# A mixture's transposes and logits put beside attention's last eight chunks, its weights given places of their own, and its other half written anew

## The reference

```python
# 1: linear attention with the delta rule; q, k, v: (4, 8, 768, 48)
for t in range(S):
    y[:, :, t] = einsum('bhd,bhde->bhe', q[:, :, t], state)
    v_old = einsum('bhde,bhd->bhe', state, k_n[:, :, t])
    state = state + beta_t * einsum('bhd,bhe->bhde', k_n[:, :, t], v_t - v_old)
x = y.transpose(0, 2, 1, 3).reshape(3072, 384)
# 2: soft mixture of 8 experts with 4 slots each
logits = x @ phi                                   # (3072, 32)
d = softmax(logits, axis=0)                        # over the tokens
slot_input = d.T @ x                               # (32, 384)
slot_out[e] = relu(slot_input[e] @ w1[e]) @ w2[e]  # w1 (8, 384, 1024), w2 (8, 1024, 384)
x = softmax(logits, axis=1) @ slot_out
# 3: feed-forward
h = x @ w_in                                       # w_in (384, 2048)
out = (h * sigmoid(1.702 * h)) @ w_out             # w_out (2048, 384)
```

## Time and profile before

| stage | from, us | to, us |
|---|---|---|
| attention, chunks 0 to 15 | 0 | 186.5 |
| attention, chunks 16 to 19 | 186.5 | 219.7 |
| attention, chunks 20 to 23 | 219.7 | 252.8 |
| transposes of x and logits | 252.8 | 291.6 |
| maxima, exponential, slots' inputs | 291.6 | 306.4 |
| experts, stacks, product with w_in | 306.4 | 360.3 |
| feed-forward | 360.3 | 590.2 |

### The profile page before, as it was taken

One profiled execution on the slowest core, in us unless ns is written; L12 is line 12 of the kernel. 1 busy time (PEld: TensorE's weight loads), 2 busy tenths in 40 slices (PEclk: granted clock), 3 DMA queues, 4 the chain that ended last, 5 costly groups with the idle time before them and its releaser, 6 DMA issues. The chain is left out here.

```text
span 590.2 us, 17597 instructions
## 1 busy us (share of the span) xinstructions
PE 488.2 (83%) x7320; PEld 354.7 (60%) x7320; DVE 364.7 (62%) x1139; ACT 281.6 (48%) x595; POOL 39.4 (7%) x50
## 2 busy tenths in 40 slices
PE   5537879788887777669898675999999999999997
PEld 4415556556554455447533323887878878788786
DVE  3997889979898981012312646655656556565563
ACT  2103765556666566612201325556555565555654
POOL 2101110110121231010000000000000000000000
PEclk9998997888998789859999987999999999999999
DMA  8401443332311511895039940001010010100101
GB/s 337 181 0 58 133 119 84 114 124 80 106 32 56 200 56 46 329 359 214 2 113 395 401 160 0 2 0 53 0 40 13 0 53 0 38 16 0 55 0 54
DMA packets 23477, 59.35 MB, mean 101 GB/s; under 512 B 2160, under 2 KB 10480, under 8 KB 23024
## 3 DMA queue, kind: packets, MB, share of 16 engines
q1 hardware_dynamic: 20768, 48.91, 23.3%
q10 hardware_dynamic: 2640, 9.44, 4.3%
HBM read 53.62 MB, written 4.72 MB: 99 GB/s over the span
## 5 line engine op out<-in xcount | busy, mean ns | idle before, releaser
L980 PE MATMUL acc<-g_h,wo_h 128*128 128x512 f32 x288 | 113.5, 394 | 5.4 <-DVE g_l L1033 3.4
L981 PE MATMUL acc<-g_h,wo_l 128*128 128x512 f32 x288 | 112.6, 391 | 0.0
L982 PE MATMUL acc<-g_l,wo_h 128*128 128x512 f32 x288 | 112.5, 391 | 0.0
L1033 DVE TENSOR_TENSOR g_l<-g,g_h 128x512 fp32r<-128x512 f32 x96 | 66.5, 692 | 72.6 <-ACT g_h L1001 72.6
L1001 ACT ACTIVATE g_h<-g 128x512 fp32r<-128x512 f32 x96 | 60.7, 633 | 79.0 <-DVE g L1030 79.0
L452 DVE TENSOR_TENSOR tmp<-nm,tt 128x110 f32<-128x110 f32 (+35 forms) x366 | 79.2, 256 | 0.4
L1030 DVE TENSOR_TENSOR g<-hp,sig 128x512 f32<-128x512 f32 x96 | 66.3, 690 | 18.9 <-ACT sig L993 11.9
L457 DVE TENSOR_TENSOR tt<-tt,tmp 128x110 f32<-128x110 f32 (+35 forms) x366 | 75.8, 247 | 0.2
L993 ACT ACTIVATE sig<-hp 128x512 f32<-128x512 f32 x96 | 57.4, 597 | 18.0 <-PE hp L962 17.7
L980 PEld LDWEIGHTS acc<-g_h,wo_h 128*128 128x128 f32 x288 | 54.4, 189 | 19.1 <-issue 3.9
L982 PEld LDWEIGHTS acc<-g_l,wo_h 128*128 128x128 f32 x288 | 54.4, 189 | 11.5
(11 more groups left out here) (132 smaller groups left out, 546.9 us busy)
## 6 DMA issues: line engine op xcount, KB each, us to landing
kq<-in_kq_t SPq DMA_DIRECT2D x24, 512.0 KB, 4.5
ring<-in_w ACTq DMA_DIRECT2D x3, 2048.0 KB, 10.0
ring<-in_w SPq DMA_DIRECT2D x3, 2048.0 KB, 12.5
ring<-in_w SPq DMA_DIRECT2D x4, 1536.0 KB, 17.0
vn<-in_v_nat SPq DMA_DIRECT2D x24, 192.0 KB, 3.7
kn<-in_k_nat SPq DMA_DIRECT2D x24, 192.0 KB, 2.4
out_t<-res SPq DMA_DIRECT2D x18, 256.0 KB, 2.1
ring<-in_w ACTq DMA_DIRECT2D x2, 1536.0 KB, 14.6
```

The costliest lines, as they stand in the source:

```text
L980: eng.matmul(acc[d][:], wo_h[:, f, cols], g_h[:, f % R], start=(f == 0), stop=False)
L981: eng.matmul(acc[d][:], wo_l[:, f, cols], g_h[:, f % R], start=False, stop=False)
L982: i = eng.matmul(acc[d][:], wo_h[:, f, cols], g_l[:, f % R], start=False, stop=(f == NF - 1))
L1033: eng.tensor_tensor(g_l[:, f % R], g[:, f % R], g_h[:, f % R].bitcast(F32), ALU.subtract).then_inc(s_gl, 1)
```

## The change

Four things are done, all in the first two parts of the program.

1. The transposes of x, the logits and their transposes back become 24 "turns", three in each of the chunks 16 to 23, in the two banks of the Gram matrices. TensorE has the turns in its order after the first `update`, after the next chunk's `ks`, and after `pz`. The copies of a turn (`turn_out`) are ACT's up to chunk 19 and DVE's from chunk 20 on. The column maximum of the first 20 tiles is taken in chunk 23 (`colp`). The identity matrix and the ones beside x are written at the start of the program by POOL, ahead of the clearing of `tt`; phi is loaded there too.
2. Slices get fixed places in one `store` (`SLICE_AT`, in KB per partition); six are issued during attention, all by SP: 0 and 1 in chunks 2 and 5, 2 in chunk 16, 3 to 5 in chunk 20, ahead of the loads for chunk 23. ACT issues none.
3. In the mixture SP issues slices 6 to 8 first, w_out behind the slots' matmuls, 9 to 11 behind the first `hidden`, 12 and 13 behind the first `out`, and w_in, now in three loads, behind the second `hidden`.
4. The mixture is written engine by engine. The transposes of the row softmax are matmuls with the identity, one per 32 output partitions (96 instead of 24), and stand before the second `hidden`. DVE's half of the relu and ACT's no longer wait for one another. All four parts of w_out are split before the second group's slots are copied out. One warm-up matmul less stands ahead of the spreading of the maximum.

The diff, cut to this. The attention part:

```diff
+        TURNS = 3
+        FIRST = NCH - NT // TURNS
+
+        def turn_out(eng, copy, s):
+
+            eng.wait_ge(p_xt, s + 1)
+            if s >= 5 and s % 4 == 1:
+                eng.wait_ge(p_lt, s // 4)
+                copy(logits[:, s - 5:s - 1], bank_x[:, DM:DM + P].rearrange("p (t s) -> p t s", s=NS)).then_inc(f_lo, 1)
+            if s >= 4:
+                eng.wait_ge(p_lg, s - 3)
+            copy(xt[:, s % 4], bank_x[:, 0:DM]).then_inc(f_x, 1)
+            if s >= 4 and s % 4 == 0:
+                eng.wait_ge(p_lg, s)
+                copy(lgt[:, s // 4 - 1], bank_l[:, 0:P]).then_inc(f_lgt, 1)
...
+            eng.dma_start(phi[:], phi_t.rearrange("(k p) s -> p k s", p=P)).then_inc(s_phi, DMA)
 
             for c in range(NCH):
+
+                if c in (2, 5):
+                    load_slice(eng, c // 3)
+                if c == NCH - 2 * CR:
+                    eng.wait_ge(p_q, NCH - 2 * CR)
+                    load_slice(eng, 2)
+                if c == NCH - CR:
+                    eng.wait_ge(p_q, NCH - CR)
+                    load_slice(eng, 3)
+                    eng.wait_ge(v_d, NR)
+                    load_slice(eng, 4)
+                    load_slice(eng, 5)
...
+            eng.memset(ident[:], 0.0).then_inc(s_pool, 1)
+            eng.wait_ge(s_pool, 2)
+            eng.affine_select(out=ident[:], in_=ident[:], compare_op=ALU.not_equal, fill=1.0, base=0,
+                              pattern=[[-1, P]], channel_multiplier=1).then_inc(s_ident, 1)
+            eng.wait_ge(s_ident, 1)
+            eng.memset(x[:, :, DM:XW], 1.0).then_inc(s_ones, 1)
...
+            def logits_of(t):
+                eng.wait_ge(f_x, t + 1)
+                if t == 0:
+                    eng.wait_ge(s_phi, DMA)
+                if t >= 4 and t % 4 == 0:
+                    eng.wait_ge(f_lgt, t // 4)
+                for k in range(KT):
+                    i = eng.matmul(bank_l[NS * (t % 4):NS * (t % 4) + NS, 0:P], phi[:, k], xt[:, t % 4, P * k:P * k + P],
+                                   start=(k == 0), stop=(k == KT - 1), skip_group_check=True)
+                i.then_inc(p_lg, 1)
+
+            def by_tokens(g):
+                eng.wait_ge(f_lgt, g + 1)
+                eng.transpose(bank_x[:, DM:DM + P], lgt[:, g], ident[:]).then_inc(p_lt, 1)
+
+            def turn(s):
+                if s:
+                    logits_of(s - 1)
+                else:
+
+                    eng.wait_ge(a_gk, NCH)
+                    eng.wait_ge(v_p, NCH)
+                    eng.wait_ge(s_ident, 1)
+                if s >= 5 and s % 4 == 1:
+                    by_tokens(s // 4 - 1)
+                eng.wait_ge(a_y, s + 1)
+                for k in range(KT):
+                    i = eng.transpose(bank_x[:, P * k:P * k + P], x[:, s, P * k:P * k + P], ident[:])
+                i.then_inc(p_xt, 1)
...
+                if late >= 0:
+                    turn(late)
...
+                if late >= 0:
+                    turn(late + 1)
...
+                if late >= 0:
+                    turn(late + 2)
+            logits_of(NT - 1)
+            by_tokens(NT // 4 - 1)
...
+                if mine:
+                    turn_out(eng, copy, late)
                 z_out(c, 1)
+                if mine:
+                    turn_out(eng, copy, late + 1)
                 s_out(c, 1)
-
-                if c == NCH - 2 * CR:
-                    eng.wait_ge(p_q, NCH - 2 * CR)
-                    load_slice(eng, 0)
-                if c == NCH - 3:
-                    eng.wait_ge(p_q, NCH - CR)
-                    load_slice(eng, 1)
-                    eng.wait_ge(v_d, NR)
-                    load_slice(eng, 3)
-                    eng.wait_ge(p_z, 2 * CR * (NR - 1))
-                    load_slice(eng, 4)
-            eng.wait_ge(p_q, NCH)
-            load_slice(eng, 2)
```

DVE, the slices and the mixture:

```diff
+                if mine:
+                    turn_out(eng, eng.tensor_copy, late)
...
+                if c == NCH - 1:
+
+                    eng.wait_ge(f_lo, NT // 4 - 1)
+                    eng.tensor_reduce(colp[:], logits[:, 0:NT - 4].rearrange("p t s -> p s t"), AX.X, ALU.max).then_inc(v_c, 1)
+                if mine:
+                    turn_out(eng, eng.tensor_copy, late + 2)
...
+            eng.wait_ge(p_lg, NT)
+            eng.tensor_copy(lgt[:, NT // 4 - 1], bank_l[:, 0:P]).then_inc(f_lgt, 1)
+            eng.wait_ge(p_lt, NT // 4)
+            eng.tensor_copy(logits[:, NT - 4:NT], bank_x[:, DM:DM + P].rearrange("p (t s) -> p t s", s=NS)).then_inc(f_lo, 1)
...
+SLICE_AT = [122, 138, 0, 16, 48, 60, 72, 28, 84, 0, 122, 134, 48, 60]
+PER = KT + NFT // FTS
...
+        eng.dma_start(slice_place(store, i), src).then_inc(s_w[i], DMA)
...
+            load_slice(eng, 6)
+            load_slice(eng, 7)
+            load_slice(eng, 8)
+            eng.wait_ge(p_slots, 1)
+            for i in range(PARTS):
+                load_w_out(i)
+
+            eng.wait_ge(p_h, KT)
+            for i in (9, 10, 11):
+                load_slice(eng, i)
+            eng.wait_ge(p_o, NFT // FTS)
+            for i in (12, 13):
+                load_slice(eng, i)
+            eng.wait_ge(p_h, 2 * KT)
+            for k in range(KT):
+                eng.dma_start(win[:, k], w_in[P * k:P * k + P]).then_inc(s_win[k], DMA)
...
+            def c_transposed(i):
+
+                if i >= 4:
+                    eng.wait_ge(v_stack, i - 3)
+                for j in range(CB):
+                    for a in range(4):
+                        m = eng.matmul(banks[i % 4][NS * a:NS * a + NS, P * j:P * j + P], cmix[:, CB * i + j], ident[:],
+                                       start=True, stop=True, skip_group_check=True)
+                m.then_inc(p_c, 1)
+
+            eng.wait_ge(v_col, 1)
+            eng.transpose(misc[0:NS, 0:P], col[:, 1], ident[:]).then_inc(p_col, 1)
+            warm_up(1)
+            eng.wait_ge(v_cdiag, 1)
+            eng.wait_ge(k_const, 2)
+            eng.matmul(banks[5][:, 0:NS], ones[:], cdiag[:], start=True, stop=True).then_inc(p_spread, 1)
...
+            hidden(0)
+            out(0)
+            eng.wait_ge(v_cmix, 1)
+            for i in range(NCB):
+                c_transposed(i)
+            hidden(1)
+            out(1)
+            eng.wait_ge(v_sot, NEG)
+            for k in range(KT):
+                eng.wait_ge(s_win[k], DMA)
+                for i in range(NMB):
+                    m = eng.matmul(banks[7][NS * i:NS * i + NS, :], so_t[:, k], win[:, k, 512 * i:512 * i + 512],
+                                   start=(k == 0), stop=(k == KT - 1), skip_group_check=True)
+            m.then_inc(p_m, 1)
```

More of the change, by code:

```diff
@@ L354, in _, with copy @@
             root(1)
+            def copy(out, src):
+                return eng.activation(out, src, ACT.Copy)
             for c in range(NCH):
-                r = c // CR + 1
+                r, late = c // CR + 1, TURNS * (c - FIRST)
+                mine = late >= 0 and c < NCH - CR
                 z_out(c, 0)
@@ L527 @@
 XW = DM + 1
-SLOTS = 5
 EG = 4
```

556 lines of the change are left out of this document (260 added, 296 removed).

## The result

Four runs of the changed kernel took 560.20 to 567.43 us, median 563.77, beside 587.00 for the kernel before; the ratio is 0.961, 95% interval 0.954 to 0.968. A second series on another chip gave 560.16 against 586.35 (first experiment). So 23 to 26 us are gained where 32 were predicted: 555 lay too low, inside its range.

A forecast was written before the change was run, and what follows sets the result against it. TensorE's transposes and logits, then transfers, bound the stages after attention. Feed-forward starting at 328.3, 32.0 earlier, gives 560.0 from the profiled 592.03, or 555.2 from the median 587.22, 4.8 lower; forecast 555, range 548 to 566.

The forecast's parts named there:

- main step: Late chunks: three turns each, 3.76 us, partly fill TensorE's idle time; a chunk takes 9.5 us instead of 6.95.
- Rivals 2 and 3: Late chunks: stretched by half clock or exposed weight loads, 566, chance 0.10; half clock there and in the tail, 600, 0.03.
- rival 5: Attention's last part or transfers: ACT, DVE or transfers were the limit all along, so the change does little; chance 0.01.
- The tail and the mixture's first half: From chunk 23's solve at 252.7: maxima 266.1, first expert matmul 278.4, output matmuls 286.1, c's transposes 292.6.
- rival 4: Mixture: c's transposes run one by one, 26.9 us instead of 5.6, giving 576; chance 0.04.
- The 1.3 us that I had set aside for half clock in the tail: End of attention: TensorE at half clock after idle time, expected to cost 1 to 2 us.
- The transfers: After attention: 20.4 MB at 388 GB/s take 52.7 us without a gap, adding 0.7 us to the path.
- rival 1: Mixture: transfers bound it, through a rate some 10% lower or a 5 us gap, giving 561; chance 0.12.
- both chains: Mixture's end: the compute path and the transfers finish within 1 us; w_in lands at 319.6, wanted at 318.9.
- the signs that I had named for being wrong: Chunks of 11 us or more, clock below 0.9, DMA waits before expert or w_in matmuls, another feed-forward length.
- attention ahead of chunk 16 was taken as unchanged: Attention before the late chunks: chunk 17's first solve stays at 195.67 us, with no added cost.
- feed-forward's 229.9 us stay: Third part of the kernel: unedited, so its length stays 229.9 us and only its start moves.

The follow-up runs named there:

- first experiment: The changed kernel and the kernel before, both unchanged, run once more with profiles; 560.16 us against 586.35, ratio 0.955.
- the second trace of the kernel before: New profile of the unchanged kernel before; profiled execution 585.39 us, span 583.6, series median 586.35 us.
- the kernel without the stall: Against the changed kernel, slices 0 and 1 are issued ahead of chunk 0 instead of in chunks 2 and 5; 556.78 us, ratio 0.951.

## Why the prediction was right, and where it was off

**Right in its main step.** The turns fill TensorE's waits as said, and what does not fit lengthens the chunk. Predicted 9.35 by the rows and 9.5 as written, measured 9.0 six times in a row, 3 us better. Chunk 21 shows where: ACT's and DVE's additional copies, which part of the added 0.15 was for, ran beside TensorE; the first turn started 2.92 us behind the solve instead of 3.01; and behind the second ks and behind pz the next group starts after 0.38 and 0.65 us, where the sum has 0.54 and 0.75, near the durations of the groups. Doubling the transposes confirmed the bound: no slack is left there. Rivals 2 and 3 (longer chunks, half clock) fall with chunks of 9.0 us and the clock of 1.00 from 200.7 to 267.6; rival 5 falls with the result.

**The tail and the mixture's first half** came within 0.5 us of their terms: solve of chunk 23 to the maxima 12.9 (13.4 predicted), to the first expert matmul 12.5 (12.3), to the output matmuls 7.75 (7.7), to c's transposes 6.5 (6.5). Those took 4.13 us for 143 instructions, 0.029 each as read from the output matmuls, so rival 4 falls; with the rest they need 5.5 us, as predicted (5.6), and 1.5 more for a stall without a releaser, behind the 143rd of the 192 instructions in ten of the eleven traces of kernels with the change. The eleventh is the kernel with doubled transposes, whose list is longer ahead of this place; there the 192 run through and 1.04 us of such a stall stand in the second hidden. The stall is of the same kind as the one in attention, below. The 1.3 us that I had set aside for half clock in the tail weren't needed there; half clock came behind it, from 268.0 to 271.4.

**The transfers** ran at 397 GB/s over 51 us, so rival 1 in its form (a lower rate) did not come. The Trainium skill, "DMA: Bandwidth & Descriptors", section Measured, has 425 GB/s for 16 MB when the pair's other core is idle; the rate here lies under that and above the per-core share that the prediction weighed and set aside. That both chains end together was read rightly: the last third of w_in landed at 322.07, as its matmuls were under way (318.83 to 323.39). Taking bytes away gained nothing, reordering DVE's work gained nothing, reordering it and bringing 2 MB forward gained 4.2 us. Of the signs that I had named for being wrong, two came: TensorE idle with "DMA" as releaser, 1.48 us ahead of the last 16 output matmuls, which cost nothing since DVE's parts ended later; and a feed-forward part of another length.

**The step that failed is the one on which no term stood: attention ahead of chunk 16 was taken as unchanged.** The late chunks are added up from 195.67, the start of chunk 17 in the trace of before, and the move of slices 0 and 1 into chunks 2 and 5 is not priced at all. In the changed kernel TensorE stalls for 3.5 us, until 8 us behind such an issue, in a chunk's solve; then runs at half clock; and chunk 17 starts 5.0 us later than in the trace of before. New stalls came with the load in chunks 12 and 14, and the one at 73 went when the load was put where TensorE waits for DVE anyhow.

The stall is a wait for TensorE's own instructions; the profile names no releaser, but its DMA packets show it. During the execution an instruction queue (q8) brings packets of 16 KB, 54 in the first trace, one for every 256 instructions in TensorE's records. In 47 such blocks in each of the fourteen traces TensorE starts a block at the earliest 1.19 us behind the end of its packet. The traces have 73 stalls without a releaser of over 0.8 us; 70 of them stand at the start of a block and end 1.3 to 1.6 us behind its packet. (The other three are one place in the experts' output matmuls of the old mixture; I have no cause for them.) A packet starts when TensorE has entered the block before: 0.7 us later (median) where the DMA engines are less than 0.3 busy in between, 2.2 us where they are more than 0.8. The place at 73, and others, from these records:

| kernel | block before entered, us | packet | next block | stall |
|---|---|---|---|---|
| after | 66.66 | 71.40 to 72.42 | 73.96 | 3.54 |
| slices 12, 13 not loaded | 65.55 | 66.45 to 67.45 | 69.27 | none |
| slices 0, 1 first | 66.09 | 67.37 to 68.33 | 69.83 | none |
| slices later, chunk 12 | 153.44 | 157.42 to 158.46 | 159.82 | 2.54 |
| before, no slice loaded | 82.57 | 86.22 to 87.18 | 88.65 | 2.15 |

So the packet that a 2 MB load holds up starts 4.0 to 4.7 us behind the block's entry, where 0.9 to 1.3 are usual at this place. With the load in chunk 2 that happened in four traces of five; in the fifth TensorE entered the block 0.62 us behind the load's issue instead of 0.85 to 0.96, and the packet went ahead of the load. The last row shows that the keys' and values' loads can do the same. In the first trace the DMA engines were full from 67 to 74 us (share 1.00), with two packets of instructions among 717. That the packet stands in line behind the load's own packets, rather than being held up in another way, is argued and not shown:

```profile
q1 hardware_dynamic: 715, 2.64, 100.4%
q8 instruction: 1, 0.02, 0.9%
q14 instruction: 1, 0.01, 0.3%
```

**The second step that failed is that feed-forward's 229.9 us stay.** They are 233.2, and 232 to 233.4 in every kernel with the change. 2.5 us of that are four starts in each group of ten that come 4 to 9 ns late. The change moved all of this part's tiles without editing a line of it; which place matters stays open.

**The sum.** Against the second trace of the kernel before (maxima at 287.77, feed-forward at 353.39), the kernel without the stall starts feed-forward at 321.92, 31.5 us earlier: nearly the 32.0 of the forecast, though by terms that partly cancel (chunks 3 us better; the trace that I subtracted from 5 us later than usual, of which 1.8 in chunk 22). Less 2.9 for the longer feed-forward, 28.6 remain, and the measured medians give 28.9. The change as it stood loses 3 to 6 more (23.2 and 26.2 gained in the two series), and the 5.0 us that the place of the two loads costs lie in that range. The offset of 4.8 between the shown trace and the median was carried over whole, which assumed that the delays of that trace would be absent from the new kernel; with the stall it got delays of its own.

## What to carry to other kernels

Work for TensorE can be put into the waits of a serial chain at full value, and its price is read from the chain's timeline to a few per cent. A large load can cost more than its bandwidth, since the instructions of a long list come through the same DMA engines: put it where the engine with that list is waiting anyway, not where the queue happens to be idle. When two chains end within a microsecond of each other, test their removal together; either one alone shows nothing, and may even lose by the clock that falls in the new wait.

## What the runs showed of the hardware that was not expected

- TensorE's instructions come during the execution, in packets of 16 KB for 256 instruction records. It stood still, with no releaser in the profile, until 1.3 to 1.6 us behind the end of such a packet in 70 stalls of 0.9 to 3.5 us.
- A 2 MB load in the middle of attention was followed, 7 to 8 us after its issue, by the end of such a stall of 2.5 to 3.5 us at each place that was tried (73.96, 73.43, 159.82, 179.48), and by clock 0.53 over the next 7 us in the first trace; but in one of five traces with the load in chunk 2 it was not (first stall 1.69 us, at 80.31).
- The spacing of matmuls with 512 columns was 226.6 to 227.3 ns at all positions in the kernel before, and for the same instructions up to 236.0 ns at four of ten positions in kernels whose tiles lie elsewhere.
- 192 instructions that write four column groups in turn, at 128 columns, took 0.029 us each; the logits' matmuls of the same width, all into one group, 0.14.
- Waits of 0.9 and 1.4 us for transfers, where there had been none, were followed by half clock over most of the next eight matmuls (5.47 us instead of 3.70).
